# Attention stage of a three-part kernel: VectorE's order in a unit changed, first keys issued from ScalarE's queue, one group of filler matmuls taken out

## What is computed

```python
scores = scale * np.matmul(q, k.transpose(0, 1, 3, 2))
mask_local = (rel >= 0) & (rel < stride)                          # heads 0 to 3
mask_strided = (rel >= 0) & (pos[None, :] % stride == pos[:, None] % stride)   # heads 4 to 7
scores = np.where(masks[None, :, :, :], scores, -1000000000.0)
scores = scores - np.max(scores, axis=-1, keepdims=True)
attn = np.exp(scores)
attn = attn / (np.sum(attn, axis=-1, keepdims=True) + 1e-09)
x = attn @ v                                                      # rows of the first expert layer
```

## Time and profile before

| what | value |
|---|---|
| median of 3 runs | 1191.69 us (1191.43 to 1191.7) |
| the profiled execution's own time | 1192.04 us |
| its span, first to last instruction | 1190.3 us |
| TensorE busy | 1163.6 us (98%) |
| mean granted TensorE clock | 0.983 |
| VectorE / ScalarE / GpSimd busy | 488.8 / 325.6 / 108.5 us |

### The profile page before, as it was taken

The page is one execution under the profiler, slowest core; times in us unless marked ns, Lnnn a source line. Parts: engine busy times, 40 slices in busy tenths (PEclk is TensorE's granted clock), DMA queues, the critical chain, the costliest instruction groups (busy, mean ns, idle before and its releaser), DMA issues.

```text
span 1190.3 us, 19136 instructions
## 1 busy us (share of the span) xinstructions
PE 1163.6 (98%) x6697; PEld 1036.0 (87%) x6697; DVE 488.8 (41%) x1003; ACT 325.6 (27%) x710; POOL 108.5 (9%) x118
## 2 busy tenths in 40 slices
PE   7999999999999999999999999999997999999997
PEld 4678999999999999999999999999896889888885
DVE  5756524214213322421421332242136556665663
ACT  5763122103112212210311221230132334343332
POOL 3222000000000000000000000000001222222221
PEclk9699999999999999999999999999998999999999
DMA  7635004002202200400220220040003676555653
GB/s 166 169 123 165 23 1 142 0 0 74 67 0 70 70 0 0 141 0 0 78 63 0 70 70 0 0 141 28 27 18 105 181 187 178 167 153 162 170 150 78
DMA packets 82337, 96.42 MB, mean 81 GB/s; under 512 B 22176, under 2 KB 56992, under 8 KB 82304
## 3 DMA queue, kind: packets, MB, share of 16 engines
q1 hardware_dynamic: 76400, 81.23, 22.9%
q0 software_dynamic: 5904, 14.75, 5.9%
HBM read 85.05 MB, written 10.91 MB: 81 GB/s over the span
## 4 chain that ended last, share of the span: by engine, by line
PE 95%; DMA 1%; DVE 1%; issue 1%; SPq 1%; ACT 1%; POOL 0%; POOLq 0%; DVEq 0%; ACTq 0%
PE bank L1161 15%; PE bank L1147 15%; PE bank L1163 15%; PE bank L1162 15%; PE bank L1149 15%; PE bank L1148 15%; PE bank L1079 1%; PE bank L1092 1%; PE bank L1371 1%; PE bank L1056 1%; DMA qkraw<-in_q_dram 1%; PE bank L1293 1%; PE bank L1356 1%; PE bank L1067 0%; PE bank L1116 0%
## 5 line engine op out<-in xcount | busy, mean ns | idle before, releaser
L1161 PE MATMUL bank<-w2hi,hhi 128*128 128x512 f32 (+1 forms) x768 | 300.9, 392 | 0.0
L1163 PE MATMUL bank<-w2hi,hlo 128*128 128x512 f32 (+1 forms) x768 | 299.8, 390 | 0.0
L1162 PE MATMUL bank<-w2lo,hhi 128*128 128x512 f32 (+1 forms) x768 | 299.7, 390 | 0.0
L1147 PE MATMUL bank<-xhi,w1hi 128*128 (+1 forms) x768 | 257.9, 336 | 2.9 <-issue 2.6
L657 ACT ACTIVATE hhi<-bank 128x384 fp32r<-128x384 f32 x184 | 90.6, 492 | 611.7 <-PE bank L1149 611.7
L1149 PE MATMUL bank<-xhi,w1lo 128*128 (+1 forms) x768 | 256.9, 335 | 0.0
L1148 PE MATMUL bank<-xlo,w1hi 128*128 (+1 forms) x768 | 256.8, 334 | 0.0
L755 DVE SCALAR_TENSOR_TENSOR hlo<-bank,hhi 128x384 fp32r<-128x384 f32 (+1 forms) x256 | 138.9, 543 | 265.7 <-ACT hhi L657 234.3
L1163 PEld LDWEIGHTS bank<-w2hi,hlo 128*128 128x128 f32 (+1 forms) x768 | 141.6, 184 | 33.1
L1162 PEld LDWEIGHTS bank<-w2lo,hhi 128*128 128x128 f32 (+1 forms) x768 | 141.7, 184 | 31.0
L1161 PEld LDWEIGHTS bank<-w2hi,hhi 128*128 128x128 f32 (+1 forms) x768 | 141.7, 184 | 30.9
(11 more groups left out here) (176 smaller groups left out, 853.8 us busy)
## 6 DMA issues: line engine op xcount, KB each, us to landing
w1raw<-in_moe_w_dram SPq DMA_DIRECT2D x68, 512.0 KB, 4.6
w2raw<-in_moe_w_dram SPq DMA_DIRECT2D x68, 512.0 KB, 4.7
qkraw<-in_q_dram SPq DMA_DIRECT2D x16, 144.0 KB
qkraw<-in_k_dram SPq DMA_DIRECT2D x16, 144.0 KB
out_dram<-ysb POOLq DMA_DIRECT2D x3, 768.0 KB
x1rows<-acc SPq DMA_DIRECT2D x9, 256.0 KB, 2.0
vloc<-in_v_dram SPq DMA_DIRECT2D x8, 144.0 KB
vstr<-in_v_dram SPq DMA_DIRECT2D x8, 144.0 KB
```

Of the source, the lines that this page charges most:

```text
L1147: pe.matmul(bank[:, 0:n], wh, xh(c), start=(c == 0), stop=False)
L1161: pe.matmul(psY[tt][0:rows, :], hh, w2hi[:, f, :], start=(f == 0), stop=False)
L1162: pe.matmul(psY[tt][0:rows, :], hh, w2lo[:, f, :], start=False, stop=False)
L1163: ins = pe.matmul(psY[tt][0:rows, :], hl, w2hi[:, f, :], start=False, stop=(f == FC - 1))
```

## The change

Four edits, no other instruction is added or taken out. (1) The two transfers of pair 0's keys are issued from ScalarE's queue, ahead of its first instruction, and no longer from SyncE's. (2) TensorE's six fillers between the transposes of the first queries and those of the first keys are gone. (3) VectorE takes `x_lo(U - 2)` ahead of unit U's maxima. (4) In units 1 to 9 VectorE copies the transposed probabilities of unit U - 1 between the maxima of head 0 and head 1; from unit 10 on the copy stays behind them.

```diff
+        def load_rows(eng, g, n, src, into):
+            b, c = g // PAIRS, g % PAIRS
+            for h in range(2):
...
+                eng.dma_start(raw, src[b, 2 * c + h].rearrange("(p t) d -> p t d", t=SP_T)).then_inc(into[g % 2], 16)
...
             def load_qk(g):
...
+                load_rows(sp, g, 0, q, q_in)
+                if g:
+                    load_rows(sp, g, 1, k, k_in)
...
+            load_rows(act, 0, 1, k, k_in)
             queries(0, 0)
...
             for U in range(UNITS):
                 rows, tiles, w = unit_shape(U)
-                for h in range(2):
-                    dve.wait_ge(scores_ready, 2 * U + h + 1)
-                    if U >= 2:
-                        dve.wait_ge(exp_ready, 2 * (U - 2) + h + 1)
-                    dve.tensor_reduce(nmax[0:rows, U % 2, h, 0:tiles], by(psS(U, h)[0:rows], w, tiles * w), AX.X, ALU.max,
-                                      negate=True).then_inc(max_ready, 1)
+                if U >= 2:
+                    x_lo(U - 2)
+                maxima(U, 0)
+                if 0 < U < FILL:
+                    probs_T(U - 1)
+                maxima(U, 1)
...
-                if U >= 2:
-                    x_lo(U - 2)
-                if U:
+                if U >= FILL:
                     probs_T(U - 1)
...
             for n in range(2):
-                if n == 1:
-                    keep_warm(WARM_FIRST, banks[0])
                 for half in range(2):
                     transpose_half(0, n, half)
```

More of the change, by code:

```diff
@@ L306, in load_w2 @@
                               ).then_inc(w2_in[u], 16)
+        def load_rows(eng, g, n, src, into):
+            b, c = g // PAIRS, g % PAIRS
+            for h in range(2):
+                raw = qkraw[g % 2][:, n, :]
+                if c < LOCAL_PAIRS:
+                    raw = raw.rearrange("p (t x) -> p t x", t=SP_T)[:, :, h * DH:(h + 1) * DH]
+                else:
+                    raw = raw.rearrange("p (h t d) -> p h t d", h=2, t=SP_T)[:, h, :, :]
+                eng.dma_start(raw, src[b, 2 * c + h].rearrange("(p t) d -> p t d", t=SP_T)).then_inc(into[g % 2], 16)
         def unit_shape(U):
@@ L314, in load_qk @@
             def load_qk(g):
-                b, c = g // PAIRS, g % PAIRS
                 if g >= 2:
                     sp.wait_ge(qk_transposed, 4 * (g - 1))
-                for n, src, into in ((0, q, q_in), (1, k, k_in)):
-                    for h in range(2):
[L320 to L328, removed]
+                load_rows(sp, g, 0, q, q_in)
+                if g:
+                    load_rows(sp, g, 1, k, k_in)
             def load_v(g):
@@ L763, in sum_parts, with maxima @@
                                   ).then_inc(lg_copied, 1)
+            def maxima(U, h):
+                rows, tiles, w = unit_shape(U)
+                dve.wait_ge(scores_ready, 2 * U + h + 1)
+                if U >= 2:
+                    dve.wait_ge(exp_ready, 2 * (U - 2) + h + 1)
+                dve.tensor_reduce(nmax[0:rows, U % 2, h, 0:tiles], by(psS(U, h)[0:rows], w, tiles * w), AX.X, ALU.max,
+                                  negate=True).then_inc(max_ready, 1)
             queries(0)
```

## The result

The changed kernel takes 1195.68 us (median of 8 runs, 1194.39 to 1196.56), the kernel before 1191.49 in the same job (8 runs, 1187.22 to 1191.7). The ratio is 1.0037, 95% interval 1.0026 to 1.0049: slower by 4.2 us, on the forecast side and inside the range of all cases, but under half of the 9.3 us of my sum and outside the forecast case's own 1198.5 to 1203. Single runs of one kernel differ by several microseconds in what follows, and two executions of the kernel before, of 1916 and 2942 us in later jobs, are counted as slow and left out throughout. The profiled execution of after has a span of 1194.8 us, that of before 1190.3.

What follows compares the result with a forecast made beforehand. TensorE was taken to bound the kernel, by its gaps and above all its clock. 8.9 us from the low clock plus 0.4 from unit 14 gave 9.3 on 1192.04, less 0.35 against the median: 1201.0 us; range over cases 1188.5 to 1203.

Steps and rivals of the forecast that it cites:

- the 9.3 us of my sum: Whole kernel: 8.9 us lost up to unit 7 at the low clock plus 0.4 from unit 14.
- forecast case: Clock falls at about 9.7 us and stays low until the logits: 1201.0 us, 1198.5 to 1203, chance 0.52.
- The clock falls when the six fillers go: Start, 6.6 to 9.7 us: without fillers TensorE is busy about 1.4 of 3.1 us, so its clock falls at about 9.7.
- Stays low until the logits: Units 1 to 6 and on: 1.2 GHz without gaps, clock back only near 73 us; unit 7's masks near 50.5 us.
- rival C: Clock falls at 9.7 us, but unit 0's six fillers restore it at about 13: 1191.5 us, 1190 to 1192.5, chance 0.10.
- the term of 8.9 us: Start to unit 7: at the low clock unit 7's masks start at 50.45 us instead of 41.55, 8.9 later.
- Worth nothing in units 1 to 9: VectorE's new order: at the low clock TensorE waits for none of it; with the clock up, a few tenths a unit, either sign.
- the signs to look for: If the clock is up, unit 5 should lose half a microsecond: `x_lo` waits behind ScalarE's weight split, and maxima behind it.
- a gain in unit 3: If the clock is up, values in unit 3 should start some 0.6 us sooner behind their scores.
- The 1.63 us of issuing: SyncE's list at the start: keys moved to ScalarE's queue bring the second queries 1.63 us earlier, 10.44 instead of 12.07.
- The sign that I had set: Start: the 1.63 us shift is wrong if the second queries land later than 10.8 us.
- The +0.4 from unit 14: Unit 14: `x_lo` first starts the maxima 0.38 us later, lengthening TensorE's 0.79 us gap; +0.4 us, bounds 0 and 0.8.

Runs made afterwards that it cites:

- e4: Kernel before without the six fillers between the first queries and the first keys, all else as before: 1192.75 us, ratio 1.0016.
- e7: Kernel before with x's low part ahead of the maxima from unit 10 on alone: 1192.01 us, ratio 0.9999.
- e1: Changed kernel with VectorE's old order, so only the keys on ScalarE's queue and the six fillers gone: 1192.34 us, ratio 1.0007.
- e2: Kernel before with VectorE's new order alone, start as before: 1195.89 us, ratio 1.0037.
- e13: Kernel before with VectorE's new order in units 1 to 3 alone: 1192.09 us, ratio 1.0011.
- e11: Changed kernel with the copy of the transposed probabilities back behind both maxima: 1192.4 us, ratio 1.0016.
- e12: Changed kernel with only the six fillers put back: 1194.46 us, ratio 1.0026.
- e14: Kernel before with VectorE's new order in units 4 to 6 alone: 1194.23 us, ratio 1.0023.
- e5: Kernel before with only the copy of the probabilities between the maxima in units 1 to 9, `x_lo` still behind them: 1198.56 us, ratio 1.0066.
- e8: Kernel before with the first keys on ScalarE's queue and the copy between the maxima in units 1 to 9: 1195.44 us, ratio 1.0035.
- e10: Changed kernel with added fillers in TensorE's waits of units 4 to 8: 1191.4 us, ratio 1.0006.
- e3: Kernel before with only the first keys' transfers moved to ScalarE's queue, all fillers kept: 1191.08 us, ratio 0.9986.
- e15: Kernel before with the first keys on ScalarE's queue, old order, six fillers kept, and added fillers in units 4 to 8: 1186.22 us, ratio 0.9954.
- e6: Kernel before with only `x_lo` ahead of the maxima in units 2 to 9: 1192.89 us, ratio 1.001.
- e9: Kernel before with three more fillers between the heads' transposed probabilities in units 4 to 8, three ahead of both in units 6 to 8: 1187.11 us, ratio 0.9975.

## Why the prediction was wrong

**The clock falls when the six fillers go: it did, but their absence is not shown to be the cause.** I had taken 9.7 us from the busy time of the stretch at 33.9 us; it fell at 7.8 in after and at 9.4 in e4, which changes nothing else. But seven of the twelve profiles that have the fillers were at the low level there too. My text also put the clock at 2.4 GHz everywhere before 37 us. As the Trainium skill has it ("TensorE: Matmul & The Clock Gate", section "What's actually happening"), throttled is the default and activity releases it. The trace of before agrees: the ten first fillers take 4.45 us, 0.44 each, and the six at 6.64 us 1.46, 0.24 each.

**"Stays low until the logits": this is the step that failed.** I carried 1.2 GHz through units 1 to 6, because in the 27 us before the logits a TensorE without gaps had not brought the clock back. It was back at 14.5 in after and at 16.1 in e4, about where unit 0's six fillers end, and nowhere later than 18.2. That was rival C, which I gave 0.10. A warning lay in rows that I used: the clock comes back a few microseconds into the logits, the first long run of full-size matmuls (128 rows, hundreds of columns), and I priced these six fillers at 2.56 us of just such work. That the fillers are what brings it back isn't shown: in e7 they ran from 13.00 to 15.77 and the clock stayed down until 18.2. So the path behind the term of 8.9 us, units 1 to 6 at the low clock, did not happen: unit 1 started at 14.83 instead of 13.93, 0.9 later, and unit 4 0.3 later; and the start edits together, measured by e1, are worth +0.9 us or nothing that can be told.

**"Worth nothing in units 1 to 9": this is the step that hid the real loss.** It hung on the step before: at a low clock TensorE has no gaps and VectorE's order can't matter. With the clock up it mattered, and e2 puts +4.4 us on the order alone, where my sum had +0.4 for all of it. I had the mechanism for unit 5 among the signs to look for (half a microsecond, `x_lo` behind the weight split: 1.17 us of VectorE's wait and 0.59 of ScalarE's), but as a small loss, and of the copy I expected a gain in unit 3. It didn't come in after: from masks to masks unit 3 takes 4.04 us, and 3.92 in before, and e13 is no faster kernel. What I missed is that the copy's source is late: in after VectorE stands idle 0.94, 0.39 and 0.82 us for it in units 2, 3 and 4. In unit 4 before, VectorE had given ScalarE both heads' maxima by 28.53, ahead of its wait for those transposes, so that wait cost nothing; in after the second maxima end at 31.05. In units 5 and 6 it is `x_lo` that waits, 1.17 and 0.48 us; with `x_lo` first and the copy behind the maxima (e11) unit 5 takes 3.95 us, with both moves (after) 4.17, and 3.49 before.

**How the 4.2 us divide: waits in part, the clock in part, and why the clock is lower stays open.** In the pair of profiles the waits of units 4 to 6 are 1.5 of the 4.5 us. Over many runs e2 can be set beside before at like mean clocks: three of its runs at 0.982 and 0.983 have a median of 1195.17 us, 55 of before 1191.60; six at 0.976 to 0.978 1197.29, and five of before 1195.95. So 1.3 to 3.6 us of the loss stay at a like clock. e2's mean clock is also lower, 0.9795 on average against 0.9832 over 125 runs of before. Within those runs 0.001 of mean clock goes with 0.66 us, so as an estimate 2.4 of e2's 4.4 us go with the clock. That the gaps of units 4 to 6 bring it down is not shown. In the profiles of e2, e12, e13 and e14 it is down by 30.4 to 31.8 us, in before at 37.0; but e13 has the old order in those units, and after, e5, e8 and e10 have the copy between the maxima there and fall at 38.4, 39.3, 47.6 and 56.7. The fall at 854 us, worth 1.6 us in the profile of after, has its like in the profiles of e1, e3, e5, e8 to e10 and e12 to e15 too, and not in those of before, e2, e4, e6, e7 and e11; that at 96.5 us is in e5 too, which has `x_lo` behind the maxima. Both go with no one edit, and I count them as chance in that pair of profiles.

**The 1.63 us of issuing: right on the issue, smaller in the end.** The second queries were issued at 6.05 instead of 7.66 and no longer waited for (e3, and after). The Trainium skill's rule ("DMA: Bandwidth & Descriptors", section "Issuing engines are not separate DMA queues", that issuing engines share the 16 DMA engines) agrees with the traces: 1.61 us of issue time was saved. But the first queries, whose keys now travel beside them, landed later: they are transposed at 6.51 to 6.93 us in seven of the eight profiles with the keys on ScalarE's queue (5.97 in e1), and at 5.28 to 5.95 in the nine others. The sign that I had set, second queries later than 10.8 us, can't be read off: TensorE got to them at 11.56 in after and 11.17 in e3 without a wait. Unit 1 came 0.9 us sooner in e3 and the total by nothing that can be told.

**The +0.4 from unit 14: right as a gap.** The gap was 1.08 us, 0.29 more than before's 0.79, and unit 14 takes 5.75 us in e7 against 5.42; but e7, with this edit alone, shows no difference in the total (0.9999), as it would have to be over 2 us to be seen.

**Still open:** how much of the loss is waits and how much clock, whether `x_lo` first in the early units costs anything (e6: 1.001, interval 0.9991 to 1.003), how often the clock falls at 30 us instead of 37, and why the new order goes with a lower mean clock.

## What to carry to other kernels

On an in-order engine, ask of every instruction that moves forward how late its input comes, and who waits for the ones that now stand behind it: a copy for which VectorE stood idle 0.44 us in unit 4 cost nothing behind both maxima, and ahead of the second ones it was part of an order that cost 0.46 us in unit 4 and 0.68 in unit 5. When a clock is forecast to fall, look just as hard for when it comes back: here it was back by 18.2 us in all twelve profiles in which it was low at the start. And where TensorE waits at 2.4 GHz, put fillers into the very waits that stand ahead of the fall: 24 of them there gave 4.4 us, while the six at the start are worth about 1.3 (e4), which is hardly clear of noise. Last, one profile of a kernel shows one draw of the clock: ask the other runs' mean clocks before a fall is put down to an edit.

## What the runs showed of the hardware

TensorE's clock isn't the same in every run of one kernel. Over the four jobs of the experiments 126 runs of before range from 1185.87 to 1199.44 us, with mean granted clocks from 0.991 down to 0.972 (and 0.931 in one); 25 of them have 0.987 or more, and their median is 1187.35 us. Of the 20 runs of after and e2 none has. With the 24 added fillers (e9) eight of twelve have. Fillers aren't the only way there: the profile of e7, with none added, is at 2.4 GHz from 18.2 to 55.6 us and has a span of 1185.9:

```profile
14.00:55.00 41.00, 33.91 (x409) 23.68 (x409) 33.09 (x86) 31.89 (x147) 14.50 (x18) 0.95 0.74 190
```

Work without gaps did not always bring the clock back. This window is of e2:

```profile
40.60:64.40 23.80, 23.80 (x168) 17.20 (x166) 16.32 (x40) 16.13 (x67) 6.74 (x8) 0.50 0.60 157
```

TensorE was busy all the time, nearly all of it with small and partial matmuls, and stayed at 1.2 GHz. Six matmuls of 512 columns on the full array, 2.42 us, stood at its return at 14.5 us in after; but in e2 itself it came back at 33.7 us, behind 3.30 us of gapless work with three such matmuls in it, so what brings it back these runs don't settle. It also fell inside dense work: at 854.3 us in after, for 3.2 us in which TensorE was busy throughout, and in eleven of the seventeen profiles near there.
